# One Sinkhorn normalization a step, its sums in PSUM, and the second product of a mixture of experts in three uneven runs

## The reference, cut to what matters

```python
logits = x @ w_gate
logits = logits - logits.max()
P = np.exp(logits)
for _ in range(8):
    P /= P.sum(1, keepdims=True) + 1e-09
    P /= P.sum(0, keepdims=True) + 1e-09
    P *= N / E
out = np.zeros((N, D), dtype=np.float32)
for e in range(E):
    h = np.maximum(x @ w1[e], 0.0)
    ye = h @ w2[e]
    out += P[:, e:e + 1] * ye
```

## Time and profile before

| | us |
|---|---|
| median of 3 runs (1627.09 to 1628.09) | 1627.23 |
| the profiled execution's own time | 1627.57 |
| its span in the trace | 1625.8 |
| PE busy | 1595.2 |
| POOL busy | 998.5 |
| DVE busy | 732.0 |
| ACT busy | 543.2 |

### The profile page before, as it was taken

The page is one execution under the profiler, slowest core; times in us unless marked ns, Lnnn a source line. Parts: engine busy times, 40 slices in busy tenths (PEclk is TensorE's granted clock), DMA queues, the critical chain, the costliest instruction groups (busy, mean ns, idle before and its releaser), DMA issues.

```text
span 1625.8 us, 24296 instructions
## 1 busy us (share of the span) xinstructions
PE 1595.2 (98%) x8880; PEld 1426.5 (88%) x8880; DVE 732.0 (45%) x1264; ACT 543.2 (33%) x774; POOL 998.5 (61%) x645
## 2 busy tenths in 40 slices
PE   7888999999999999999999999999999999999999
PEld 6877888888898888889888898888889888898888
DVE  5757634434434434434434344344344344344343
ACT  4742232332323333233232332334323333233331
POOL 5975555656556777565656656677565655656552
PEclk9999999999999999999999999999999999999999
DMA  7611212122121213212112121122211212122111
GB/s 216 180 54 52 74 56 78 52 77 75 54 77 52 77 52 117 78 52 78 65 64 77 52 77 63 66 77 91 78 62 68 78 52 77 57 72 77 52 65 39
DMA packets 34157, 120.41 MB, mean 74 GB/s; under 512 B 3904, under 2 KB 4160, under 8 KB 34112
## 3 DMA queue, kind: packets, MB, share of 16 engines
q1 hardware_dynamic: 34112, 119.80, 21.5%
HBM read 115.06 MB, written 4.72 MB: 74 GB/s over the span
## 4 chain that ended last, share of the span: by engine, by line
PE 94%; POOL 3%; DVE 2%; issue 1%; ACT 0%; POOLq 0%; DVEq 0%
PE ps L456 17%; PE ps L455 16%; PE ps L457 16%; PE ps L439 14%; PE ps L435 14%; PE ps L437 14%; POOL probs L756 1%; POOL sc L748 1%; PE ps L356 0%; PE ps L345 0%; PE ps L333 0%; DVE prob L1010 0%; DVE row_sum L985 0%; PE ps L502 0%; POOL t_raw L737 0%
## 5 line engine op out<-in xcount | busy, mean ns | idle before, releaser
L714 POOL TENSOR_TENSOR w_lo<-w_raw,w_hi 128x1792 fp32r<-128x1792 f32 (+2 forms) x98 | 391.0, 3990 | 529.5 <-ACT w_hi L548 529.4
L597 ACT ACTIVATE h_hi<-ps 128x384 fp32r<-128x384 f32 x384 | 189.0, 492 | 961.8 <-DVE ps L887 450.3
L456 PE MATMUL ps<-w_lo,h_hi 128*128 128x512 f32 x1152 | 457.0, 397 | 0.0
L457 PE MATMUL ps<-w_hi,h_lo 128*128 128x512 f32 x1152 | 456.6, 396 | 0.0
L455 PE MATMUL ps<-w_hi,h_hi 128*128 128x512 f32 x1152 | 455.3, 395 | 1.3 <-POOL w_lo L721 1.3
L439 PE MATMUL ps<-xv_hi,w_lo 128*128 128x384 f32 x1344 | 452.6, 337 | 0.0
L435 PE MATMUL ps<-xv_hi,w_hi 128*128 128x384 f32 x1344 | 450.8, 335 | 1.4 <-DVE logits L965 1.4
L437 PE MATMUL ps<-xv_lo,w_hi 128*128 128x384 f32 x1344 | 450.0, 335 | 0.0
L869 DVE SCALAR_TENSOR_TENSOR h_lo<-ps,h_hi 128x384 fp32r<-128x384 f32 x384 | 214.1, 558 | 361.6 <-ACT h_hi L597 360.9
L435 PEld LDWEIGHTS ps<-xv_hi,w_hi 128*128 128x128 f32 x1344 | 253.3, 188 | 31.4 <-DVE logits L965 1.5
L437 PEld LDWEIGHTS ps<-xv_lo,w_hi 128*128 128x128 f32 x1344 | 253.2, 188 | 29.1
(11 more groups left out here) (75 smaller groups left out, 948.1 us busy)
## 6 DMA issues: line engine op xcount, KB each, us to landing
w_raw<-w SPq DMA_DIRECT2D x192, 512.0 KB, 3.9
qk_buf<-qk SPq DMA_DIRECT2D x16, 576.0 KB, 5.5
v_win<-v SPq DMA_DIRECT2D x16, 288.0 KB, 4.3
out<-x_raw SPq DMA_DIRECT2D x18, 256.0 KB, 2.6
const_sb<-consts SPq DMA_DIRECT2D x1, 176.0 KB, 3.5
wg<-w_gate SPq DMA_DIRECT2D x1, 64.0 KB, 4.3
```

Of the source, the lines that this page charges most:

```text
L456: nc.tensor.matmul(ps_y[t], h_hi[slot][:, f, c], w2_lo[slot][:, f, :], start=False, stop=False)
L457: last = nc.tensor.matmul(ps_y[t], h_lo[slot][:, f, c], w2_hi[slot][:, f, :], start=False, stop=closes)
L597: nc.scalar.activation(h_hi[slot][:, f, half * HT:(half + 1) * HT], o, ACT.Relu)\
L714: last = nc.gpsimd.tensor_tensor(w1_lo[:, slot, c], w1_raw[:, slot, (lo + 1) * BLK:(hi + 1) * BLK], w1_hi[:, slot, c].bitcast(F32), ALU.su ...
```

## The change

**Runs of the second product.** The seven places now hold the halves `(0, 0), (0, 0), (0, 0), (0, 2), (2, 2), (2, 11), (11, 12)`: P1, P6, P2 and P7 follow each other without a half between them, then come 2 halves, P5 and P4, 9 halves, P3, 1 half.

**Sinkhorn.** Steps 1 to 8 hold one round each. The matmul for the columns stands after P4; its result is read after rest 2, followed by the next round's rows. The sums and inverses are kept in PSUM, in the unused ends of the two banks. Window 8 computes the last product of the eighth round, and PE waits for it before step 9. Steps 4 to 11 are written out for this, instead of a loop.

**Expert 0 of block 0** is taken raw (a copy on DVE), since its weights aren't known yet. ACT multiplies the six tiles by their weights in step 8, between relu_21 and relu_12; DVE's take of expert 1 waits for each.

**The maximum.** ACT makes the diagonal matrix, DVE negates the maximum, and ACT's exponential adds it as a bias, so that the logits are not shifted. PE no longer waits for the logits before step 1 but before the first half of the last token tile in step 1. DVE's order within a step is new: c22, c21, rest 1, rest 2 in place of c22, rest 1, c21, rest 2, and takes 1 to 4 stand just before c12.

```diff
+RUNS = [(0, 0), (0, 0), (0, 0), (0, 2), (2, 2), (2, 11), (11, 12)]
...
-        row_sum = sb(ctx, "row_sum", [P, NT])
-        row_inv = sb(ctx, "row_inv", [P, NT])
...
+        col_sum = [a[:, 0:E] for a in spread]
+        col_inv = [a[:, E:2 * E] for a in spread]
+        row_sum = [a[:, 2 * E:2 * E + NT] for a in spread]
+        row_inv = [a[:, 2 * E + NT:2 * E + 2 * NT] for a in spread]
...
+                if isinstance(n, int) and n == 0 and t == TT - 1 and f == 0:
+                    pe.wait_ge(logits_out, 1)
...
-                for k, (lo, hi) in enumerate([(0, 2), (2, 4), (4, 6), (6, 8), (8, 10), (10, 11), (11, 12)]):
+                for k, (lo, hi) in enumerate(RUNS):
+                    if columns and k == P1:
+
+                        pe.wait_ge(col_part_ready, columns + 1)
                     if top and k == P7:
                         pe.wait_ge(max_all_ready, 1)
...
+                    if top and k == P4:
+                        pe.wait_ge(col_part_ready, 1)
                     multiply(s, first, n, slot, k)
...
+                    if columns is not None and k == P4:
+                        spread_columns(columns, 1 - slot)
...
-            pe.wait_ge(logits_out, 1)
...
+            def max_spread_out():
+                act.wait_ge(max_part_out, 1)
+                nc.scalar.activation(max_diag[:], ident, ACT.Copy, scale=max_part[:, 0:1]).then_inc(max_part_ready, 1)
+
+            def weigh_first():
+
+                act.wait_ge(chain, SINKHORN * 8)
+                for t in range(TT):
+                    act.wait_ge(y_taken, t + 1)
+                    o = acc[:, 0, t * DM:(t + 1) * DM]
+                    at = place(0, t)
+                    nc.scalar.activation(o, o, ACT.Copy, scale=prob[:, at, 0:1]).then_inc(first_weighed, 1)
...
                 relu_21(n, slot)
+                if isinstance(n, int) and n == SINKHORN:
+                    weigh_first()
                 relu_12(n, slot)
...
+            max_spread_out()
             w2_split(16, 0, 0)
...
                 add_u2(n, slot)
                 if top:
-                    shift_logits(1 - slot)
...
+                    read_max(1 - slot)
...
                 add_c22(n, slot)
+                if sinkhorn is not None:
+                    dve.wait_ge(col_sum_ready, sinkhorn + 1)
+                add_c21(n, slot)
                 rest(n, slot, bank[slot], 1, 1, 1)
...
                 rest(n, slot, bank[1 - slot], 1, 0, 2)
+                if sinkhorn is not None:
+                    columns(sinkhorn, 1 - slot)
+                    if not final:
+                        row_sums(sinkhorn + 1, 1 - slot)
+                        rows(sinkhorn + 1, 1 - slot)
+                some(0 if final else 1, 5)
                 add_c12(n, slot)
```

More of the change, by code:

```diff
@@ L470, in spread_columns, with window @@
                 pe.wait_ge(col_part_ready, i + 1)
-                nc.tensor.matmul(spread[at][:, 0:E], ones[:], col_part[:], start=True, stop=True)\
+                nc.tensor.matmul(col_sum[at], ones[:], col_part[:], start=True, stop=True)\
                   .then_inc(col_sum_ready, 1)
-            def window(s, first, n, j, taken, top=False, after_p6=None, after_p7=None, after_p4=None):
+            def window(s, first, n, j, taken, top=False, columns=None):
                 halves = [(t, f) for t in range(TT) for f in range(2)]
                 slot = j % 2
-                for k, (lo, hi) in enumerate([(0, 2), (2, 4), (4, 6), (6, 8), (8, 10), (10, 11), (11, 12)]):
+                for k, (lo, hi) in enumerate(RUNS):
+                    if columns and k == P1:
+                        pe.wait_ge(col_part_ready, columns + 1)
                     if top and k == P7:
                         pe.wait_ge(max_all_ready, 1)
[L483 to L486, removed]
+                    if top and k == P4:
+                        pe.wait_ge(col_part_ready, 1)
                     multiply(s, first, n, slot, k)
@@ L523, in _ @@
                     n = s * PER_SB + j
[L524 to L534 removed]
+                    if n:
+                        window(s, j == 0, n, j, None if n == 1 else n // FP * TT - 2 * TT, n == 1,
+                               n - 1 if n <= SINKHORN else None)
+                if s == 0:
+                    for n in range(FP, 3 * FP):
+                        if n == SINKHORN + 1:
+                            pe.wait_ge(chain, SINKHORN * 8)
+                        window(s, False, n, n % FP, n // FP * TT - (2 * TT if n % FP == 0 else TT), False,
+                               n - 1 if n <= SINKHORN else None)
+                with pe.Fori(1 if s else 3, E) as e:
                     for j in range(FP):
@@ L681, in _ @@
                         window(n, landed(n), j)
-                with act.Fori(1, E - 1) as e:
+                if s == 0:
+                    for n in range(FP, 3 * FP):
+                        window(n, landed(n), n % FP)
+                with act.Fori(1 if s else 3, E - 1) as e:
                     for j in range(FP):
@@ L899, in take @@
                 dve.wait_ge(y_done, done + (t + 1))
+                if s == 0 and isinstance(e, int) and e == 1:
+                    dve.wait_ge(first_weighed, t + 1)
                 o = acc[:, s, t * DM:(t + 1) * DM]
@@ L903, in take @@
                 weight = flat[:, at:at + 1] if isinstance(at, int) else flat[:, bass.ds(at, 1)]
-                if first:
+                if first and s == 0:
+                    nc.vector.tensor_copy(o, ps_y[t]).then_inc(y_taken, 1)
+                elif first:
                     nc.vector.tensor_scalar(o, ps_y[t], weight, None, ALU.mult).then_inc(y_taken, 1)
@@ L907, in take, with window @@
                     nc.vector.scalar_tensor_tensor(o, ps_y[t], weight, o, ALU.mult, ALU.add).then_inc(y_taken, 1)
-            def window(n, j, takes=None, top=False, after_p6=None, after_p7=None, after_p4=None):
+            def window(n, j, takes=None, top=False, sinkhorn=None):
                 slot = j % 2
-                last = after_p6 == SINKHORN - 1
+                final = sinkhorn == SINKHORN - 1
                 def some(lo, hi):
@@ L919, in some @@
                             take(*takes[:3], t, takes[3])
-                if after_p6 is not None:
-                    dve.wait_ge(col_sum_ready, after_p6 + 1)
                 if top:
```

107 lines of the change are left out of this document (34 added, 73 removed).

## The result

The changed kernel takes 1642.98 us (median of 4 runs, 1641.96 to 1644.09); the kernel before took 1627.32 beside it. The ratio is 1.0096, with a 95% interval of 1.0078 to 1.0113: slower by 1%, 15.7 us. Predicted were 1638.6 us and a range from 1631 to 1649.

The account below looks back on a forecast made before the run. PE, busy 98% of the span, was taken to set the end. Step 1 +1.8, steps 2 to 4 -12.1, 5 to 8 +1.7, 9 to 95 +17.4, 32 and 64 +2.6: +11.4 onto 1627.2 gives 1638.6 us, range 1631 to 1649.

Parts of the forecast that it names:

- What bounds it: Whole kernel: PE, busy 98% of the span, sets the end at 15.66 us a step; Sinkhorn costs 18.3 at the start.
- P6 comes too early: Each steady step: P6 waits for rest 3, 0.14 late plus 0.17 for release and bare weight load, +0.31 us.
- the weight load is hidden across the wait: Rival at P6's wait: 0.20 in place of 0.31 us a step, total 1628.6, no change; chance 0.08.
- lateness alone: Rival at P6: only rest 3's 0.14 counts, +0.03 us a step, total 1623, faster; chance 0.05.
- Longer runs: Second product's halves in each steady step: fewer starts of 512-column runs save time, -0.11 us a step.
- Runs don't help: Rival on the halves: only columns set a matmul's turn, step 15.97, total 1649; chance 0.12.
- steps 9 to 95: Term for the 87 steps after Sinkhorn's: net +0.20 us each, +17.4 in all.
- The room of 0.02: P7's wait for add_u2: 1.19 us with release and load, against 1.21 that P2 covers, so just in time.
- P7 is late as well: Rival at P7's wait for add_u2: its release costs 0.1 more a step, 9 us, total 1648; chance 0.07.
- Steps 32 and 64: P5 waits for rest 0, as relu_11 stands behind w1_split in ACT's order: 1.3 us twice, +2.6.
- Steps 2 to 4: One Sinkhorn round a step ends PE's waits for DVE: 48.2 us where before took 60.3, -12.1.
- Step 1: ACT's diagonal delays rest 0, P5 stands still for 4 us, the clock drops; step 2 begins 1.8 us later.

Follow-up runs that it names:

- the half more: The changed kernel with 8 halves behind P4 and 2 behind P3 in place of 9 and 1: 1616.73 us, ratio 0.9933.
- the cut: The changed kernel with halves in four runs of 2, 2, 6 and 2 behind P7, P5, P4 and P3: 1621.82 us, ratio 0.9961.
- the last experiment: The changed kernel with DVE's loops written out and nothing else: 1639.91 us, ratio 1.0069.
- the first experiment: The changed kernel with the second product's seven runs of the kernel before: 1712.25 us, ratio 1.0514 from three of its four runs.
- The second experiment: The kernel before with the new runs and the changed kernel's order of takes, c21 and rests on DVE: 1668.88 us, ratio 1.0253.

## Why the prediction held, point by point

The direction and the range held, and the time was 4.4 us too low. The main mechanism was right; in step 1 two misses cancelled, which was luck.

- **What bounds it** (right): PE alone from start to start, and the first four steps. Nothing of DVE's 35 us less was seen in the time.
- **P6 comes too early** (right, and the largest term): predicted +0.31 a step, 0.30 on the trace, and the half more took 0.30 away. The second matmul 0.28 behind the first, as was said. The rival "the weight load is hidden across the wait" is out: the load that waits began 0.05 after the rest's end, P3's in the earlier trace rows and P6's in after alike. The Trainium skill (TensorE: Matmul & The Clock Gate, Step-by-step: what each phase is for) has loads pulled ahead of running matmuls, and these rows show that this doesn't reach across such a wait. The rival on the faster side, lateness alone, is out for the same reason.
- **Longer runs** (right): -0.11 predicted, 0.09 to 0.10 by the half more (its runs are one half less long), 0.033 a start by the cut. "Runs don't help" is out.
- **Steady step in the loops** (mis-sized, the largest miss): the term "steps 9 to 95" was 87 x 0.20 = 17.4. Outside the loops the step took 15.867 where 15.86 was said, which makes 0.6 over 87 steps; in the loops it took 0.02 to 0.07 more still, 2.9 us over the 67 steps, and 3.1 by the last experiment. The start of add_u2 at 0.46 was right. The room of 0.02 was worked out against the matmul's turn (1.21 behind P6's last start), and that turn was kept. But the load's own place in the stream is 0.17 before it, at 1.04, and the load came at 1.07. The rival "P7 is late as well" had named the place, though not this mechanism, and at 9 us it was three times too dear.
- **Steps 32 and 64** (right in mechanism, a little large): 2.6 predicted, 1.10 twice. The wait is gone when relu comes first.
- **Steps 2 to 4** (right): -12.1 predicted, -12.0. Each takes 16.10 to 16.12 where 16.08 was said. The row sums in PSUM never took over 0.185.
- **Step 1** (right in mechanism, near in number by luck): P5 waited 3.89 (4 predicted) and began 11.2 into the step, as was said, though the diagonal took 0.40 (0.25 to 0.3 predicted). The start of step 1 was -0.2 in place of -1.5, and that isn't a miss that the runs can size: in the kernels here that have the diagonal first it lies from 106.5 to 109.8. Against these 1.3 stands a term that was too large: from P5 to step 2 the trace has 131.03 - 119.24 = 11.8, the prediction 12.7. It added the lower clock (some 1.5, a price that no row gave) to P4's wait for DVE's first rows. On the trace the two overlap: at the lower clock P5 itself took 2.09 (119.24 to 121.33), and DVE's rows were done at 121.19, so P4 hardly waited. The two misses leave 0.4.
- **Not predicted**: that the rest of the change isn't neutral under the old runs (the first experiment, 94 us above its expectation). The prediction didn't need it. But the new order of rest 1 and c21 costs nothing only with enough halves between P4 and P3. The second experiment's expectation was too low for a like reason: it didn't count the halves that had covered the rounds.

So the change is two gains and three losses. The gains are 15 us by the new router (12 in steps 2 to 4 and, once P5 doesn't wait, 20.6 - 17.4 = 3 in step 1, with the sums in PSUM as a part of it) and 9 us by long runs. The losses are 28 us at P6, 8 by ACT's order in steps 1, 32 and 64, and 3 by DVE's loop at P7; the spreading matmul in steps 5 to 8 costs 1 more. The balance is 28 + 8 + 3 + 1 - 15 - 9 = 16, where 15.7 were measured. These are rounded shares: the 12 are net of P6's wait and the long runs in the same three steps, which is 0.6. Within the router's gain, one round a step, the maximum without the wait for the logits, and expert 0 taken raw were not tried apart. Each of the three losses could be taken away without giving up a gain, and then 1603.3 are left where before had 1627.3 to 1628.7.

## What to carry to other kernels

When work is moved together into one long run, write down for each wait of the engine what now stands between the last thing that feeds the wait and the wait itself, and compare it with the length of that chain (here 2.06 us against 1.92). What such a miss costs isn't only the difference: here a matmul released by another engine also paid for its release and for a weight load that nothing hid (0.17 together), so a room of less than that was none. And when a list of one engine is in a fixed order, put what somebody waits for before what is merely due (relu before the weights, rest before the sum that waits for PE).

## What the runs showed of the hardware

- In a stream of matmuls of 512 columns, each with its own weight load, the distance settled at 0.227 after nine, in the last run of before as in the middle of a step of after; one more start of such a run behind 384 columns cost 0.033 (a step of 15.600 in place of 15.567).
- A weight load that came 0.03 late cost up to 0.07 in the step, more than its lateness, and no matmul's own row shows a wait: the six matmuls of P7 together took 0.03 longer, and the six of the two halves behind them 0.04.
- An operation of DVE in a loop started 0.46 behind the matmul that it waits for, written out 0.37. PE's loops cost nothing that could be measured.
- A DVE operation on 18 numbers a partition with its operands in SBUF took from 0.18 to 2.42; the 2.42 lasted until the POOL instruction beside it ended. With its operands in PSUM it took 0.184 to 0.185 all eight times.
